# Experts' first product as seven block products (one level of Strassen, in Winograd's form) instead of eight, in a three-part kernel on one core

## The reference

```python
# 1 attention, 2 x 8 heads, 576 tokens, 64 wide: local softmax part and a memory part, mixed by a gate -> x (1152 x 512)
# 2 dense layer pair
h = x @ w_in                                   # 512 -> 2048
g = np.maximum(h, 0.0) + np.log1p(np.exp(-np.abs(h)))
x = g @ w_out                                  # 2048 -> 512
# 3 eight experts, every token goes through each of them
logits = x @ w_gate; P = np.exp(logits - logits.max())
for _ in range(8):                             # the balancing loop
    P /= P.sum(1, keepdims=True) + 1e-09
    P /= P.sum(0, keepdims=True) + 1e-09
    P *= N / E
for e in range(E):
    h = np.maximum(x @ w1[e], 0.0)             # 512 -> 1024, the "first product"
    ye = h @ w2[e]                             # 1024 -> 512
    out += P[:, e:e + 1] * ye
```

## Time and profile before

| | us |
|---|---|
| median of 3 runs (1195.54 to 1196.05) | 1195.59 |
| span of the profiled execution | 1193.6 |
| TensorE busy in it | 1165.9 |
| VectorE busy | 475.2 |
| ScalarE busy | 412.1 |
| GpSimd busy | 119.1 |

### The profile page before, as it was taken

The page is one execution under the profiler, slowest core; times in us unless marked ns, Lnnn a source line. Parts: engine busy times, 40 slices in busy tenths (PEclk is TensorE's granted clock), DMA queues, the critical chain, the costliest instruction groups (busy, mean ns, idle before and its releaser), DMA issues.

```text
span 1193.6 us, 19356 instructions
## 1 busy us (share of the span) xinstructions
PE 1165.9 (98%) x6549; PEld 1062.2 (89%) x6549; DVE 475.2 (40%) x1044; ACT 412.1 (35%) x982; POOL 119.1 (10%) x215
## 2 busy tenths in 40 slices
PE   4899999999999999999999999999999999999998
PEld 3777789999999999999999999999999999999997
DVE  4888964354346154313411421331241242133111
ACT  3788766576666113212311311221131131122110
POOL 4877730000000000000000000000000000000000
PEclk9999999999999999999999999999999999999999
DMA  3612112003002100300210030030012003000000
GB/s 71 198 39 66 33 71 72 0 1 142 0 0 103 39 1 1 141 1 1 102 39 0 27 114 0 0 141 0 0 70 70 0 0 141 0 0 0 27 27 27
DMA packets 49064, 52.72 MB, mean 44 GB/s; under 512 B 31488, under 2 KB 32512, under 8 KB 49024
## 3 DMA queue, kind: packets, MB, share of 16 engines
q1 hardware_dynamic: 49024, 52.20, 13.2%
HBM read 49.83 MB, written 2.36 MB: 44 GB/s over the span
## 4 chain that ended last, share of the span: by engine, by line
PE 93%; issue 3%; DVE 2%; POOL 1%; ACT 0%; DVEq 0%; POOLq 0%; ACTq 0%
PE ps_h L1064 43%; PE ps_y L1064 42%; PE ps_o L1064 3%; PE ps_s L1064 2%; PE ps_p L1093 1%; PE ps_o L1105 1%; POOL prob L447 1%; PE ps_g L1064 1%; DVE xl L732 0%; PE ps_t L1045 0%; DVE negmax L789 0%; DVE nrm L768 0%; DVE nrm_e L772 0%; DVE ptl L732 0%; PE ps_s L1083 0%
## 5 line engine op out<-in xcount | busy, mean ns | idle before, releaser
L878 DVE SCALAR_TENSOR_TENSOR hl<-ps_h,hh 128x384 fp32r<-128x384 f32 x192 | 107.1, 558 | 565.7 <-ACT hh L637 565.7
L637 ACT ACTIVATE hh<-ps_h 128x384 fp32r<-128x384 f32 x192 | 94.4, 492 | 635.3 <-PE ps_h L1064 635.3
L1064 PE MATMUL ps_h<-yh,w1h 128*128 128x384 f32 x768 | 260.5, 339 | 0.0
L1064 PE MATMUL ps_h<-yh,w1l 128*128 128x384 f32 x768 | 260.1, 339 | 0.0
L1064 PE MATMUL ps_h<-yl,w1h 128*128 128x384 f32 x768 | 259.4, 338 | 0.0
L1064 PE MATMUL ps_y<-w2h,hl 128*128 128x512 f32 x576 | 227.0, 394 | 0.0
L1064 PE MATMUL ps_y<-w2l,hh 128*128 128x512 f32 x576 | 226.9, 394 | 0.0
L1064 PE MATMUL ps_y<-w2h,hh 128*128 128x512 f32 x576 | 225.6, 392 | 0.0
L1064 PEld LDWEIGHTS ps_h<-yl,w1h 128*128 128x128 f32 x768 | 144.1, 188 | 8.8
L1064 PEld LDWEIGHTS ps_h<-yh,w1h 128*128 128x128 f32 x768 | 144.1, 188 | 7.8
L1064 PEld LDWEIGHTS ps_h<-yh,w1l 128*128 128x128 f32 x768 | 144.5, 188 | 0.0
(11 more groups left out here) (153 smaller groups left out, 1519.6 us busy)
## 6 DMA issues: line engine op xcount, KB each, us to landing
raw<-in_moe_w_dram SPq DMA_DIRECT2D x16, 2048.0 KB, 7.9
raw<-in_moe_w_in_dram SPq DMA_DIRECT2D x2, 2048.0 KB, 8.0
raw<-in_moe_w_out_dram SPq DMA_DIRECT2D x2, 2048.0 KB, 11.3
out_dram<-acc SPq DMA_DIRECT2D x9, 256.0 KB, 2.2
q_nat<-in_q_dram SPq DMA_DIRECT2D x16, 128.0 KB, 2.4
k_nat<-in_k_dram SPq DMA_DIRECT2D x16, 128.0 KB, 2.5
v_nat<-in_v_dram SPq DMA_DIRECT2D x16, 128.0 KB, 2.4
z_nat<-in_z_prev_dram SPq DMA_DIRECT2D x8, 64.0 KB, 2.9
```

The source lines that it names most:

```text
L637: act.activation(hh[:, slot % RING, :], ps_h[:, slot % 2, 0:N2], ACT.Relu).then_inc(h_hi, 1)
L878: dve.scalar_tensor_tensor(out=hl[:, slot % RING, :], in0=ps_h[:, slot % 2, 0:N2], scalar=0.0, in1=hh[:, slot % RING, :].bitcast(F32), op0 ...
L1064: last = pe.matmul(dst, a[x], b[y], start=start and i == 0, stop=stop and i == 2)
```

## The change

Stages 1 and 2 keep their matmuls. In stage 3 an expert is cut into two halves of 512 hidden features (s counts halves, 16 in all), and a half into four units u = 0 to 3 (U = 4 s + u). A unit has 256 features (pair i = u % 2) and half of the tokens' blocks: u = 0, 1 are tokens 0 to 511 (blocks of NA = 256), u = 2, 3 are tokens 512 to 1151 (blocks of NB = 320). The unit's product is a 2 by 2 by 2 block product (256 features, 512 inputs, 2 token blocks), made of seven block products P1 to P7 of two input tiles each, so 7 x 2 x 3 = 42 matmuls of 256 or 320 columns. Their operands need four sums of weight blocks and four of token blocks, made on GpSimd (`weight_sums` once for each s and pair, `token_sums` once for each token block pair), and each of the seven operands is split in high and low. The results need seven additions: five by VectorE from PSUM (`sum_u2`, `sum_u3`, `result_11`, `sum_12`, `result_21`), two by GpSimd (`result_22`, `result_12`), and two plain copies by ScalarE (`take_s1`, `take_p5`). The relu, as before, is split by ScalarE (`relu_hi`) and VectorE (`relu_lo`), now from four SBUF tiles `h11` to `h22`.

The second product keeps its matmuls (T0 to T3 or T4: one tile of 128 tokens, 6 matmuls of 512 columns). It adds over the two pairs of a half and is then drained, so 9 drains of 512 columns for each half, 18 for each expert. TensorE runs the seven products of the next unit between the T tiles of this one, in the order P1 P6 P5 T0 P2 P7 T1 P3 T2 P4 T3 T4. "Loop u" below is this sequence with the T tiles of unit u.

Weights come in quarters of an expert into a ring of two places for w1 and two for w2 (`load_c`). The logits are 16 unsplit float32 matmuls of 288 columns, issued as soon as `y1` is complete; the balancing loop is spread over loops 0 and 1 of the first half (`SUMS`), and T0 of unit 2 waits for its end. All tiles are placed by address, with the new ones over space that stages 1 and 2 no longer use.

```diff
+    NSUB = 2 * E
+    NA, NB = 256, (T - 512) // 2
+    TA, TB = 2 * NA // P, 2 * NB // P
+    ZT = TA + TB
...
+        bank_a, bank_b, bank_c = ps_h[:, 0, :], ps_g[:, 0, :], ps_h[:, 1, :]
+        bank_sk = ps_g[:, 1, :]
+        PROD = {"P1": (0, 0), "P6": (4, 4), "P5": (3, 3), "P2": (1, 1), "P7": (5, 5), "P3": (6, 2), "P4": (2, 6)}
+        PLACE = {"P1": 1, "P6": 2, "P5": 3, "P2": 4, "P7": 5, "P3": 6, "P4": 7}
+        BANK = {"P1": bank_a, "P2": bank_a, "P6": bank_b, "P7": bank_b, "P4": bank_b, "P5": bank_c, "P3": bank_c}
...
+            def load_c(fp, place, w1, w2, waits):
+                if waits:
+                    sp.wait_ge(c1_lo, 2 * fp - 2)
+                    sp.wait_ge(c1_sum, 4 * fp - 4)
+                sp.dma_start(rc1[place][:, :, :, :].rearrange("p k f c -> p k (f c)"), w1).then_inc(ld_c1[place], 16)
+                if waits:
+                    sp.wait_ge(c2_lo, fp - 1)
+                sp.dma_start(rc2[place][:, :, :], w2).then_inc(ld_c2[place], 16)
...
+            def token_sums(t0, n, sums, done):
+                b11, b12 = y1[:, 0:2, t0:t0 + n], y1[:, 0:2, t0 + n:t0 + 2 * n]
+                b21, b22 = y1[:, 2:4, t0:t0 + n], y1[:, 2:4, t0 + n:t0 + 2 * n]
+                pool.tensor_tensor(sums[:, 0, :, :], b12, b11, ALU.subtract).then_inc(done, 1)
+                pool.wait_ge(done, 1)
+                pool.tensor_tensor(sums[:, 1, :, :], b22, sums[:, 0, :, :], ALU.subtract).then_inc(done, 1)
+                pool.wait_ge(done, 2)
+                pool.tensor_tensor(sums[:, 3, :, :], b21, sums[:, 1, :, :], ALU.subtract).then_inc(done, 1)
+                pool.tensor_tensor(sums[:, 2, :, :], b22, b12, ALU.subtract).then_inc(done, 1)
+            def weight_sums(s, i):
+                fp = 2 * s + i
+                pool.wait_ge(ld_c1[i], 16 * s + 16)
+                if not (isinstance(fp, int) and fp == 0):
+                    pool.wait_ge(c1_los, fp)
+                a11, a12 = rc1[i][:, 0:2, 0, :], rc1[i][:, 2:4, 0, :]
+                a21, a22 = rc1[i][:, 0:2, 1, :], rc1[i][:, 2:4, 1, :]
+                pool.tensor_tensor(ws[:, 0, :, :], a21, a22, ALU.add).then_inc(c1_sum, 1)
+                pool.tensor_tensor(ws[:, 2, :, :], a11, a21, ALU.subtract).then_inc(c1_sum, 1)
+                pool.wait_ge(c1_sum, 4 * fp + 1)
+                pool.tensor_tensor(ws[:, 1, :, :], ws[:, 0, :, :], a11, ALU.subtract).then_inc(c1_sum, 1)
+                pool.wait_ge(c1_sum, 4 * fp + 3)
+                pool.tensor_tensor(ws[:, 3, :, :], a12, ws[:, 1, :, :], ALU.subtract).then_inc(c1_sum, 1)
+            def weight_sums_lo(fp, i):
+                pool.wait_ge(c1_hi, 3 * fp + 3)
+                pool.tensor_tensor(w1c_l[i][:, 3:7, :, :], ws[:, :, :, :], w1c_h[i][:, 3:7, :, :].bitcast(F32),
+                                   ALU.subtract).then_inc(c1_los, 1)
+            def result_22(U, u):
+                n = width(u)
+                pool.wait_ge(p5_done, U + 1)
+                pool.wait_ge(u3_done, U + 1)
+                pool.tensor_tensor(h22[:, 0:n], u3[:, 0:n], p5[:, 0:n], ALU.add).then_inc(h22_done, 1)
+            def result_12(U, u):
+                n = width(u)
+                pool.wait_ge(t12_done, U + 1)
+                pool.tensor_tensor(h12[:, 0:n], h12[:, 0:n], p5[:, 0:n], ALU.add).then_inc(h12_done, 1)
+            pool.wait_ge(y_drained, KT * (C1 + 2) + KT)
+            token_sums(0, NA, xas, xa_sum)
+            weight_sums(0, 0)
+            weight_sums_lo(0, 0)
+            weight_sums(0, 1)
+            result_22(0, 0)
+            result_12(0, 0)
+            weight_sums_lo(1, 1)
+            pool.wait_ge(y_drained, KT * G1 * C1 + KT)
+            token_sums(2 * NA, NB, xbs, xb_sum)
...
+            def expert(e, last):
+                for half in range(2):
+                    s, final = 2 * e + half, last and half == 1
+                    for u in range(4):
+                        U = 4 * s + u
+                        if not (final and u == 3):
+                            result_22(U + 1, (u + 1) % 4)
+                            result_12(U + 1, (u + 1) % 4)
+                        if u == 1 and not final:
+                            weight_sums(s + 1, 0)
+                        elif u == 2 and not final:
+                            weight_sums_lo(2 * s + 2, 0)
+                            weight_sums(s + 1, 1)
+                        elif u == 3 and not final:
...
+                        if new:
+                            act.wait_ge(prod, 7 * U + 7)
+                            weights_hi(s + 1, u % 2, 0)
+                        take_s1(V, v)
+                        if new:
+                            weights_hi(s + 1, u % 2, 1)
+                        take_p5(V, v)
+                        if new:
+                            weights_hi(s + 1, u % 2, 2)
+                        relu_hi(V, v, "11")
+                        if u == 3 and not final:
+                            act.wait_ge(unit_done, U)
+                            weights2_hi(s + 1, 0)
+                        if u == 0:
+                            if not start:
+                                act.wait_ge(unit_done, U)
+                            weights2_hi(s, 1)
+                        if start and u == 0:
+                            act.wait_ge(g_max, 3)
+                            act.activation(weight[:, :, :].rearrange("p t e -> p (t e)"), bank_sk[:, 0:NTT * E], ACT.Exp,
+                                           bias=sk_max[:, 2:3]).then_inc(g_exp, 1)
+                        relu_hi(V, v, "22")
+                        relu_hi(V, v, "12")
+                        relu_hi(V, v, "21")
...
-            def relu_lo(n, slot):
-                dve.wait_ge(h_hi, n + 1)
-                dve.scalar_tensor_tensor(out=hl[:, slot % RING, :], in0=ps_h[:, slot % 2, 0:N2], scalar=0.0,
-                                         in1=hh[:, slot % RING, :].bitcast(F32), op0=ALU.max, op1=ALU.subtract)\
-                    .then_inc(h_lo, 1)
...
+            def sum_u2(U, u):
+                n = width(u)
+                dve.wait_ge(s1_done, U + 1)
+                dve.wait_ge(prod, 7 * U + PLACE["P6"])
+                dve.tensor_tensor(u2[:, 0:n], bank_b[:, 0:n], s1[:, 0:n], ALU.add).then_inc(u2_done, 1)
...
+            def relu_lo(U, u, quarter):
+                n = width(u)
+                dve.wait_ge(e_hi, 4 * U + QUARTER[quarter] + 1)
+                rows = {"11": h11, "22": h22, "12": h12, "21": h21}[quarter]
+                dve.scalar_tensor_tensor(out=z_place(u, quarter, 1), in0=rows[:, 0:n], scalar=0.0,
+                                         in1=z_place(u, quarter, 0).bitcast(F32), op0=ALU.max, op1=ALU.subtract)\
+                    .then_inc(e_lo, 1)
...
+                        if new:
+                            weights_lo(2 * s + u, u % 2, 0)
+                        sum_u2(V, v)
+                        if new:
+                            weights_lo(2 * s + u, u % 2, 1)
...
+                        if drains:
+                            drain_z(e, half, u, 0, first)
+                        result_11(V, v)
+                        sum_u3(V, v)
+                        relu_lo(V, v, "11")
...
+                        if u == 3 and not final:
+                            weights2_lo(2 * s + 2, 0)
+                        if u == 0:
+                            weights2_lo(2 * s + 1, 1)
...
+                        if drains:
+                            drain_z(e, half, u, 1, first)
+                        sum_12(V, v)
+                        relu_lo(V, v, "22")
...
+                        result_21(V, v)
+                        relu_lo(V, v, "12")
...
+                        if drains:
+                            drain_z(e, half, u, 2, first)
+                        relu_lo(V, v, "21")
...
+            def hidden2(s, u, names):
+                U, n, i = 4 * s + u, width(u), u % 2
+                start = isinstance(s, int) and s == 0
+                xh_, xl_ = (xah, xal) if u < 2 else (xbh, xbl)
+                for name in names:
+                    w, x = PROD[name]
...
+                    if u < 2:
+                        if w >= 3:
+                            pe.wait_ge(c1_los, 2 * s + i + 1)
+                        else:
+                            pe.wait_ge(c1_lo, 4 * s + 2 * i + (2 if w == 2 else 1))
...
+                    elif name == "P1":
+                        pe.wait_ge(h11_done, U)
+                    elif name == "P6":
+                        pe.wait_ge(h21_done, U)
+                    elif name == "P5":
+                        pe.wait_ge(t12_done, U)
+                    if name == "P2":
+                        pe.wait_ge(s1_done, U + 1)
+                    elif name == "P7":
+                        pe.wait_ge(u2_done, U + 1)
+                    elif name == "P3":
+                        pe.wait_ge(p5_done, U + 1)
+                    elif name == "P4":
+                        pe.wait_ge(u3_done, U + 1)
```

(90 more changed lines are left out.)

671 lines of the change are left out of this document (400 added, 271 removed).

## The result

| | us |
|---|---|
| before, median of 4 runs (1195.54 to 1196.05) | 1195.67 |
| after, median of 4 runs (1159.04 to 1161.71) | 1160.12 |
| ratio, with its 95% interval | 0.970 (0.969 to 0.972) |
| span of the profiled execution after | 1159.6 |

The change makes the kernel 3.0% faster. The page of after, which answers to the earlier trace rows: more instructions, VectorE's share up from 40% to 63%, GpSimd's from 10% to 38%, and a dip in PE and in PEclk in slices 14 and 15.

The account below looks back on a forecast made before the run. TensorE's issue of columns was taken to bound stage 3. Terms: 1193.6 - 50 + 2 + 12 + 5 = 1162.6 us of span, the median 2.0 over it, say 1165 us; own range 1153 to 1177, with rivals 1149 to 1190.

Parts of the forecast that it names:

- the forecast case: Whole kernel: the summed terms hold, about 1165 us, own range 1153 to 1177; chance 54%.
- Product saving, 50 us: Stage 3: seven block products instead of eight save 50 us, bounds 29 to 54, with a half at 47.0 us.
- The rival at 0.133 us: Stage 3: 256 columns don't run at 0.117 us in long runs but at stage 2's spacing; 1182 us, chance 10%.
- Logits, +2: Logits: 16 unsplit matmuls of 288 columns replace 36 split ones, 8.9 us at most against 6.4; +2 us (0 to 2.5).
- Steady loops, +5: Stage 3's steady loops: GpSimd and VectorE sharing SBUF costs 0.3 us each half, 5 us (0 to 24).
- The lock: SBUF: a VectorE instruction with two SBUF inputs and a GpSimd instruction reading SBUF exclude each other; the later one blocks.
- The handovers: Steady loops: unseen register work for waits and who goes first eat the spare time; 0.3 us for each half.
- Start of stage 3, 12 us: First loops of stage 3: token sums and the balancing loop move onto the path; 12 us (5 to 20).
- The maximum and its way through GpSimd and ScalarE (1.3): Start of stage 3, in VectorE's work for loops 0 and 1: the balancing loop's maximum takes 1.3 us.
- Everything hides: Rival, stage 3: full 54 us saved, start only 5 us, no lock cost; 1149 us, chance 10%.
- GpSimd keeping the lock: Rival, steady loops: VectorE never gets in between GpSimd's chained weight sums, 1.5 us a half; 1184 us, chance 18%.
- Slower than before: Rival, steady loops: same lock, GpSimd's strided weight sums longer than 2.1 ns for each element; 1224 us, chance 7%.

Follow-up runs that it names:

- the kernel with the eighth product: Against the changed kernel, block product P2 of every unit issued twice, so eight block products a unit again: 1212.2 us, ratio to before 1.013.
- the kernel with the late maximum: Changed kernel with rounds spread over loops 0 to 5, maximum on TensorE behind T1 and T2, sum_u2 and round 5 earlier: 1148.45 us, best of the study.
- the kernel without the maximum: Against the changed kernel, GpSimd's maximum over the partitions left out, each partition using its own: 1156.4 us, ratio 0.967.
- the kernel with three additions: Against the changed kernel, three further GpSimd additions of two SBUF tiles behind weight_sums_lo in loops 2 and 3 of each half: 1172.6 us, ratio 0.981.
- the kernel with six additions: Against the changed kernel, six further GpSimd additions of two SBUF tiles behind weight_sums_lo in loops 2 and 3 of each half: 1218.1 us, ratio 1.019.

## Why the prediction was right, and where it was not

The median came 5 us under the 1165 forecast and inside its range; the forecast case was the one that happened. By its steps:

- **Product saving, 50 us: right.** Spacings 0.119 and 0.146 us for 0.117 and 0.147, a half 47.2 us for 47.0. Sixteen halves of 50.4 before and 47.2 after differ by 51 us; the kernel with the eighth product gives the same by another way. The rival at 0.133 us is out.
- **Logits, +2: right.** TensorE's first start behind them is 7.86 us after their own first, before 6.28: +1.6. An unsplit matmul of 288 columns takes 0.49 us, not the 0.55 of the bound.
- **Steady loops, +5: too much, it was 0.** The lock is there: `relu_lo` took 0.68 us on average (L1163, 172.1 us for 256) where it is about 0.42 to 0.48 alone. But the last one ends at 501.31 and T0 starts at 502.21, 0.9 us to spare for the 0.5 counted; `weight_sums_lo` ends at 500.04 and P6 starts at 500.77, 0.7 for 0.3. The handovers that I charged 0.3 us for cost nothing. VectorE works 63 us in 100, 30 a half, where I had counted 23, too little even beside the lock; it had room for that too. That the margin is this thin was right: 4.6 us more of GpSimd work a half cost 0.8, and 9.2 cost 3.6.
- **Start of stage 3, 12 us: too little, about 15.** Two ways agree. Idle time is 11.7 us, and starts that stand wider than their steady spacing make 6.0, of which 2.8 remain at full clock in the kernel with the late maximum: 11.7 + 3.2 = 14.9. And that kernel's span is 12.5 us shorter with 2.7 of its own waits left: 15.2. Within it, the P7 wait for `sum_u2` was 1.6 (0 to 2 predicted), the waits for column sums 10.1 in four places (8 in six, and 2 for the lock). Two things were not in the sum: the half-clock behind waits, about 3 us, and GpSimd's stillness on both sides of its maximum.
- **"The maximum and its way through GpSimd and ScalarE (1.3)" is the step that failed.** From VectorE's reduction at 392.80 to the first balancing row at 397.09 (order of time, VectorE and ScalarE, below) it took 4.3 us. GpSimd began 1.5 us after the reduction's end, and ScalarE's exponential (L924) 1.6 us after VectorE had the negated maximum at 395.12, because `relu_hi` and a copy of w2 stand ahead of it in ScalarE's order (the same 1.6 us in the kernel without the maximum). And the 7.1 us behind the maximum delayed `result_22`. I took the path as it was before, with the 0.38 us of the instruction's row as GpSimd's price. There the MODIFY_POOL_CONFIG records lay 200 us earlier, and no instruction stood behind the maximum on GpSimd, so neither side could be seen; it should have been a bound. Without the maximum 3.7 us go.

```profile
392.80 0.22 DVE L1303 TENSOR_REDUCE sk_max<-ps_g 128x1 f32<-128x72 f32 x1
394.97 0.15 DVE L1305 TENSOR_SCALAR sk_max<-sk_max 128x1 f32<-128x1 f32 x1 [1.95 <-POOL sk_max L603]
...
396.75 0.30 ACT L924 ACTIVATE weight<-ps_g,sk_max 128x72 f32<-128x72 f32 x1
...
397.09 0.23 DVE L1239 TENSOR_REDUCE sk_row<-weight 128x9 f32<-128x72 f32 x1 [0.73 <-ACT weight L924]
```

- **The rivals.** Everything hides (1149) is out for this kernel by its start of stage 3; the kernel with the late maximum comes to 1148.45 once most of that is gone. GpSimd keeping the lock (1184): the kernel with three additions shows VectorE getting in after a single instruction, which cost it 0.45 us. The rule of the Trainium skill ("SBUF — State Buffer", Who interferes with whom) holds for one instruction against one, as in the swollen `relu_lo`; it does not build up over a chain in these traces. Slower than before (1224) is of the right kind: with 9.2 us more for GpSimd a half the kernel is 1.9% slower than before, but through program order and P6, and not through the lock.

With the real terms: 1193.6 - 51 + 1.6 + 15 + 0 = 1159.2 us of span, against 1159.6. The two errors, +5 in the loops and -3 at the start, had opposite signs; that the sum came as near as 3 us was in part luck. One sum of the chances is wrong: 54%, 18%, 10% and half of 10% are 87%, not 82%, for the range of 1149 to 1190. The profiled execution took 1161.7 us, 2.1 over its span as assumed; the median of the four stands 1.6 lower.

## What to carry to other kernels

The stage whose bound engine has no hole gave back what was taken from its columns in full (51 us of 51 by columns), because in the steady loops every other engine's chain was laid out against the new program order; the places to look are the start of the stage and the first loops, where one-time work (splits, a normalization) stands in the same queues. Read margins from the trace after: a loop without a wait can still be 0.7 us from one, and a wait of 2.0 us on TensorE cost 1.6 more in clock (3.6 a half in the kernel with six additions). An instruction that is moved to where its engine has something to do next must be priced with what follows it, not by the duration of its row.

## What the runs showed that I had not expected

GpSimd needs time on both sides of the maximum over the partitions: 5.6 to 6.0 us before it, put down to "issue" and mostly hidden while it had nothing to do, and 7.0 to 7.1 us after it, before the next ordinary instruction (three kernels). The records ahead of both are MODIFY_POOL_CONFIG. Where they lay long before, in the kernel before, nothing of the first part was left. The Trainium skill ("GPSIMD Engine Reference", 2.1 Instruction dispatch) puts about 6 us on the first call of freshly loaded code; the rows agree with that for the maximum, and show that the way back took as much or more. With the maximum left out neither appears.

The granted clock fell behind waits of 2 to 3 us (0.67 over the next 4 us, 0.53 over 2 us in the kernel with six additions), with matmul starts 1.8 times as far apart, and did not behind the waits of 1.47 and 1.62 us in the kernel after and of 1.25 us in the last kernel. Which lengths of wait it needs was not tried.

Left open: whether the waits left in the best kernel (by starts, 1.4 us for a round's `weight` at 403 us, 0.6 at 400 and 0.8 at 480 us) can go too, and how much of the four `weight_sums` could move to VectorE's spare time without a new wait.
